# Moving steps between the slots of a hand-written order: attention steps, xr's splits, x2's splits and weight pieces

## The reference

```python
# attention, batch 8, heads 8, seq 576, head_dim 64, 32 packed queries
p_packed = softmax(p @ k.T / 8) @ v
x = softmax(q @ p_packed.T / 8) @ p_packed        # laid out as (8, 576, 512)
# first mixing layer, d_model 512, d_ff 1024
xk = mu_k * x + (1 - mu_k) * x_prev
xr = mu_r * x + (1 - mu_r) * x_prev
x2 = sigmoid(xr @ w_r) * (relu(xk @ w_k) ** 2 @ w_v)
# second mixing layer, rank 32, 4 * d_model = 2048
u = x2 + (x2.T @ U @ V).T
out = u + relu(u @ w_ch1) @ w_ch2
```

## Time and profile before

| what | us |
|---|---|
| median of 3 runs | 1340.4 (1338.31 to 1340.59) |
| the profiled execution | 1340.01 |
| its span | 1338.2 |
| TensorE busy | 1304.4 |
| VectorE busy | 957.9 |
| ScalarE busy | 697.1 |
| GpSimd busy | 233.5 |

### The profile page before, as it was taken

The page is one execution under the profiler, slowest core; times in us unless marked ns, Lnnn a source line. Parts: engine busy times, 40 slices in busy tenths (PEclk is TensorE's granted clock), DMA queues, the critical chain, the costliest instruction groups (busy, mean ns, idle before and its releaser), DMA issues.

```text
span 1338.2 us, 21378 instructions
## 1 busy us (share of the span) xinstructions
PE 1304.4 (97%) x7626; PEld 1128.1 (84%) x7626; DVE 957.9 (72%) x1557; ACT 697.1 (52%) x1233; POOL 233.5 (17%) x328
## 2 busy tenths in 40 slices
PE   7899999999999999999999999999999999999997
PEld 6768888878888888888999999888888888888886
DVE  5977978786878777774568676857587566857557
ACT  4657556456555555544546554645355534645353
POOL 3702132324142103511002003000030003000000
PEclk9999999999999999999999999999999999999999
DMA  9646595839384614965888899787757886678766
GB/s 241 160 76 107 124 177 128 161 101 175 81 173 106 156 24 123 286 189 132 276 271 253 271 267 314 237 248 218 233 187 197 258 225 213 192 207 215 220 194 136
DMA packets 431577, 252.57 MB, mean 189 GB/s; under 512 B 311536, under 2 KB 350480, under 8 KB 431472
## 3 DMA queue, kind: packets, MB, share of 16 engines
q1 hardware_dynamic: 414768, 232.31, 65.4%
q0 software_dynamic: 10096, 17.78, 4.9%
q10 hardware_dynamic: 6608, 1.11, 0.5%
HBM read 201.25 MB, written 49.81 MB: 188 GB/s over the span
## 4 chain that ended last, share of the span: by engine, by line
PE 75%; DVE 5%; SPq 4%; DMA 3%; issue 1%; ACT 1%; POOL 0%; DVEq 0%; ACTq 0%
PE bank L1178 25%; PE bank L1264 24%; PE bank L923 9%; PE bank L909 8%; PE bank L888 5%; SPq L1450 2%; DMA w_ring<-w_parts 1%; SPq L1588 1%; PE bank L1005 1%; PE bank L1077 1%; PE bank L713 1%; DMA kq_parts<-in_q 0%; DMA x_scratch<-x 0%; DVE square L972 0%; DVE x2s_lo L1016 0%
## 5 line engine op out<-in xcount | busy, mean ns | idle before, releaser
L1178 PE MATMUL bank<-u_parts,w_ring 128*128 128x512 f32 (+1 forms) x1680 | 353.7, 368 | 1.1 <-DVE hid_raw L1223 1.1
L1264 PE MATMUL bank<-hid_parts,w_ring 128*128 128x512 f32 (+1 forms) x1680 | 349.5, 368 | 1.2 <-DVE acc L1312 0.5
L1264 PEld LDWEIGHTS bank<-hid_parts,w_ring 128*128 128x128 f32 x1680 | 304.9, 188 | 44.2 <-issue 3.8
L1178 PEld LDWEIGHTS bank<-u_parts,w_ring 128*128 128x128 f32 x1680 | 304.9, 188 | 40.9 <-issue 1.8
L1287 ACT ACTIVATE hid_parts<-hid_raw 128x512 fp32r<-128x512 f32 (+1 forms) x280 | 164.7, 588 | 134.6 <-PE bank L1264 133.8
L1293 DVE TENSOR_TENSOR hid_parts<-hid_raw,hid_parts 128x512 fp32r<-128x512 f32 (+1 forms) x280 | 180.8, 646 | 63.5 <-ACT hid_parts L1287 59.0
L909 PE MATMUL bank<-xk_hi,wk_hi 128*128 128x384 f32 x384 | 132.1, 344 | 1.9 <-DVE x L983 1.9
L909 PE MATMUL bank<-xk_lo,wk_hi 128*128 128x384 f32 x384 | 129.5, 337 | 0.0
L909 PE MATMUL bank<-xk_hi,wk_lo 128*128 128x384 f32 x384 | 129.3, 337 | 0.0
L923 PE MATMUL bank<-wv_hi,k_hi 128*128 128x512 f32 x288 | 113.5, 394 | 0.0
L923 PE MATMUL bank<-wv_lo,k_hi 128*128 128x512 f32 x288 | 112.2, 390 | 0.0
(11 more groups left out here) (176 smaller groups left out, 1937.1 us busy)
## 6 DMA issues: line engine op xcount, KB each, us to landing
w_ring<-w_parts SPq DMA_DIRECT2D x560, 256.0 KB, 3.7
w_parts<-early_out SPq DMA_DIRECT2D x23, 896.0 KB, 5.0
x_scratch<-x SPq DMA_DIRECT2D x144, 64.0 KB, 2.1
kq_parts<-in_q SPq DMA_DIRECT2D x112, 72.0 KB, 2.9
w_parts<-piece_out SPq DMA_DIRECT2D x9, 896.0 KB, 4.6
kq_parts<-in_k SPq DMA_DIRECT2D x96, 72.0 KB, 4.0
x_tiles<-x_scratch SPq DMA_DIRECT2D x6, 1024.0 KB, 6.7
v_rows<-in_v POOLq DMA_DIRECT2D x41, 128.0 KB, 5.6
```

Of the source, the lines that this page charges most:

```text
L1178: last = nc.tensor.matmul(to, wring[:, e % RW, ct, a, :], uc[:, pos, b, ct, 0:w], start=(pos in FRESH and ct == 0 and a == 0 and b == 0), ...
L1264: last = nc.tensor.matmul(role(st, j, BANK_OF[pos])[:, 0:w], wring[:, e % RW, j, a, :], hid[:, no % RH, b, 0:w], start=(pos in FRESH and i ...
```

## The change

- FIRST_AT and EARLY_AT: early pieces move from 31, 38, 43 to 33, 39, 44 in the first group, and from 35, 39 to 36, 41 in the two middle groups.
- The batch whose plan is named fourth: norm1 from 50 to 51 and outA from 53 to 54 everywhere; pp from 40 to 41 and scores2 from 42 to 43 in the middle groups. Slot 51 is slot 0 of the next group, so norm1 comes to lie behind the chunk's border.
- Batch 1 in C0: pv and qA from slot 4 to 5, qB from 5 to 6.
- x2's split of slot 0 is placed ahead of the k tile's item instead of behind it. For TensorE nothing is changed by that; ScalarE and VectorE do the split before they wait for k0.
- xr's splits of the second and third chunk of a group (C2, C4, C5, C7, C8, C10, C11) move from slot 14 of the chunk before to slot 3 of their own chunk. C1 had its split at slot 4 of its own, and C0, C3, C6, C9 at slot 3 of their own, and keep it.
- In the last group the first four loads of pieces (ws_load) move from slot 6 to slot 4.

```diff
--- before.py
+++ after.py
@@ -69,7 +69,7 @@
 NG, NU = 2, 4
 NPROD = 7
 PIECES = 2 * 2 * NG * NU
-EARLY, FIRST_AT, EARLY_AT = 20, (23, 31, 38, 43), (1, 6, 11, 15, 27, 31, 35, 39)
+EARLY, FIRST_AT, EARLY_AT = 20, (23, 33, 39, 44), (1, 6, 11, 15, 27, 31, 36, 41)
 SLOTS_P = 3
 RW, RH = 11, 3
 MIX_AT = (9, 10, 12, 14)
@@ -100,14 +100,14 @@
 
     if kind == FIRST:
         third = batch_slots(15, 17, 20, 22, 23, 24, 25, 26, 28, 29, 31, 35, 36)
-        fourth = batch_slots(37, 38, 40, 42, 43, 44, 45, 46, 47, 49, 50, 53, 55)
+        fourth = batch_slots(37, 38, 40, 42, 43, 44, 45, 46, 47, 49, 51, 54, 55)
     else:
         third = batch_slots(6, 8, 11, 13, 15, 16, 17, 19, 21, 23, 25, 28, 30)
-        fourth = batch_slots(32, 33, 35, 37, 38, 39, 40, 42, 45, 47, 50, 53, 55)
+        fourth = batch_slots(32, 33, 35, 37, 38, 39, 41, 43, 45, 47, 51, 54, 55)
     here = (3, {at: steps for at, steps in fourth.items() if at < CHUNKS * NSLOT})
     rest = (1, {at - CHUNKS * NSLOT: steps for at, steps in fourth.items() if at >= CHUNKS * NSLOT})
     if kind == FIRST:
-        second = {0: ("scores1",), 2: ("a",), 4: ("pv", "qA"), 5: ("qB",), 8: ("pp",), 9: ("scores2",),
+        second = {0: ("scores1",), 2: ("a",), 5: ("pv", "qA"), 6: ("qB",), 8: ("pp",), 9: ("scores2",),
                   10: ("sm1", "norm0"), 11: ("norm1",), 13: ("outA",), 14: ("outB",)}
         return [(1, second), (2, third), here]
     return [rest, (2, third), here] if kind == MIDDLE else [rest]
@@ -133,14 +133,14 @@
     last_chunk = kind == LAST and c == CHUNKS - 1
     for at, slot in enumerate(SLOTS):
         s = c * NSLOT + at
+        if at == 0 and (c > 0 or kind != FIRST):
+            items.append(("x2s", 7 if c == 0 else 3 * c - 2, -1 if c == 0 else 0))
         items.append(slot)
         if at == (5 if c == 2 else 3) and (c > 0 or kind != FIRST):
             items.append(("x2s", 3 * c - 1, 0) if c > 0 else ("x2s", 8, -1))
         if c > 0 or kind != FIRST:
             behind = -1 if c == 0 else 0
-            if at == 0:
-                items.append(("x2s", 7 if c == 0 else 3 * c - 2, behind))
-            elif at == 2:
+            if at == 2:
                 items.append(("g", 7, 1, -1) if c == 0 else ("g", 3 * c - 2, 0, 0))
                 if c == 2:
                     items.append(("g_evac", 0, 0))
@@ -160,14 +160,14 @@
             items.append(("g", 3 * c, int(c == 2), 0))
         if not last_chunk:
 
-            at0 = (15, 15) if kind == FIRST and c == 0 else MIX_AT if c < 2 else MIX_AT[:3]
+            at0 = (15, 15) if kind == FIRST and c == 0 else MIX_AT[:3]
             for where, one in zip(at0, (("mix", 0), ("split", 0), ("mix", 1), ("split", 1))):
                 if at == where:
                     items.append(one + (c + 1,))
         if kind == FIRST and c == 1 and at in (2, 4):
             items.append(("mix" if at == 2 else "split", 1, 1))
-        if kind != FIRST and c == 0 and at == 3:
-            items.append(("split", 1, 0))
+        if at == 3 and (kind != FIRST or c == 2):
+            items.append(("split", 1, c))
         if kind == FIRST and c == 0 and at in (1, 3):
             items.append(("mix" if at == 1 else "split", 1, 0))
         if kind == FIRST and c == 0 and at in (2, 4):
@@ -223,7 +223,7 @@
 def piece_items():
 
 
-    plan = {6: [("ws_load", EARLY + m) for m in range(SLOTS_P + 1)]}
+    plan = {4: [("ws_load", EARLY + m) for m in range(SLOTS_P + 1)]}
     for m in range(PIECES - EARLY):
         n, at = EARLY + m, 9 + 9 * m // 5
         if 0 < m < PIECES - EARLY - SLOTS_P:
```

## The result

The changed kernel is slower. Its time is 1341.0 us (median of 20 runs) against 1338.4 for the kernel before in the runs beside it; the ratio is 1.0025, 95% interval 1.0016 to 1.0034, which is 2 to 4.5 us. The forecast was 1338.4 on a time before of 1340.4, a ratio of 0.9985.

A forecast was written before the change was run, and what follows sets the result against it. TensorE was taken to bound the kernel, busy 97% of the span, with its first-phase waits to win. The chunk terms summed to -1.85 us, giving 1338.2 or 1338.6, stated as 1338.4; range 1334.5 to 1342, to hold 8 in 10.

The forecast's parts named there:

- C4 and C7: Middle chunks: the split in slot 3, ahead of sm1, delays k5's relu and r0 by 0.55 each; +1.1 us, bounds 0 and +3.6.
- C10 and C11: Last group: the split delays relu5 in C10 and the sums for the u matmul in C11, 0.5 each; +1.0 us.
- the C10 wait of 1.1 stays: Expected in the profile after: TensorE's wait of 1.1 us in C10 remains.
- C2: First group: the 1.88 wait for x and probably the half rate go, new waits take some back; -1.9 us.
- C3: x2's low part goes ahead of k0, removing a 0.84 wait, but outA's copy comes later for outB; 0 us.
- C6 and C9: The same reorder of x2's split, norm1 and outA where no wait was: +0.2 and +0.05; bounds 0 and +1.5.
- C5 and C8: pp one slot later, behind k7, so its 1.27 wait for packed goes; -1.4 us each, -2.8 together.
- C0: pv behind k5 loses its 1.42 wait, but relu5 holds r0 and scores2 comes up to 0.5 later; +0.5 us.
- Rival 4: New waits in front of outB in C2 and C3 tip TensorE's clock to half rate: 1341.5 us, chance 0.05.
- rival 2: The slot 3 split delays TensorE in full in C4, C7, C10, C11; C5 and C8 gain 0: +5.95, 1346; chance 0.15.
- three signs of being wrong: No L888 wait in C4 and C7; L689 still waiting in C5; C0's pv wait coming back as gain at 73.50.

The follow-up runs named there:

- scores2 without outA: The kernel with pp and scores2 one slot later in C5 and C8, plus C0's scores2, sm1, norm0 and norm1 one slot later: 0.9992 of the kernel before.
- the one with a single line of it: The kernel before with only pp and scores2 one slot later in C5 and C8 (40 to 41, 42 to 43): ratio 0.9963, 1332.8 us.
- C0 alone: The kernel before with only batch 1's pv, qA and qB one slot later in C0: ratio 1.0014.
- the last one: The changed kernel without the moves of xr's splits and without C0's moves: ratio 0.9979 of the kernel before, 1334.3 us.

## Why the prediction was wrong

The step that failed is the price of the splits' arrival. The prediction has for C4 and C7 "Slots 8 to 13 follow with slack. +1.1", and for C10 and C11 "+1.0". Measured between the two profiles: +2.9 and +2.4, and close to it in the kernel with the splits alone (+2.7 and +2.0). The first wait was as worked out with the earlier trace rows: r0 was to start 0.55 later, and starts 0.53 later in both. What I did not follow was the same delay one bank further: norm0 and k7's square on VectorE, then k7's high part and the sigmoid's table load on ScalarE, stand between the split and r0's evacuation, and v0 wants that bank. So the sum lacks a term that it put at nothing ("with slack"): TensorE idles 0.44 and 0.58 more in front of v0, and with the first matmuls behind each wait 0.9 and 1.0 come on top of the 0.53. In C10 the relu was 0.95 late, not 0.5, and the wait on x2s_lo, of which the prediction says that "the C10 wait of 1.1 stays", grew to 1.70. It is 1.2 to 1.7 in the four kernels with C10's split in slot 1 or 3 and 0.6 to 1.1 in the eight others. In the three with slot 3 ScalarE stood 3.9 to 4.4 for GpSimd's sum, in those eight 3.4 to 3.7; why is open. In C11 the wait for the sums grew by 0.8, not 0.5.

The other steps, in the prediction's order:

- C2: forecast -1.9, found -1.4. The 1.88 wait and the half rate went; the new waits stood where they were put: outB on L823 (forecast 1.1, found 0.87) and scores1 on the key transposes (forecast 0.7, found 1.13). The splits alone gave -1.8 there. Part of it is the state of the one execution: with the old order and full rate C2 is 53.0, not 53.8. So the end of the half rate is worth 0.8 by itself, and not the 1.65 of its matmuls, since at full rate outB waits 0.68 for its copy.
- C3: forecast 0, found -0.2; the wait at outB was forecast at 1.3 and is 0.81. Right.
- C6 and C9: +0.25 forecast, +0.8 found in this pair. Over the six kernels with this reorder C6 is 0.2 to 0.8 longer and C9 0.1. Right in kind, too small for this pair.
- C5 and C8: -2.8 forecast, -3.0 found. VectorE's packed began at 315.60 in C5 and pp at 316.93, without a wait. Right.
- C0: +0.5 forecast, +1.0 found, and +1.3 between the means of the four kernels with the new order (54.7 to 57.2) and the seven with the old (54.3 to 55.9), which overlap. The wait in front of r0 was named, but I let it end there: the clock fell behind it, and r0's 12 matmuls took 4.4 us instead of 2.8. Rival 4 had the mechanism, at the wrong places.

The sum of the forecast's chunks was -1.85, found +2.6 from the phase's first k tile on; of the 4.4 us between them 3.2 are the four chunks of the splits. So rival 2's mechanism decided it in the four chunks, at 5.3 of the 7.1 us that it had for them. Its total of +5.95 was more than twice the +2.6 found, mostly since C5 and C8, which it let gain nothing, kept their 3.0. The range of 1334.5 to 1342 held the time itself, and that was luck: the kernel before took 1338.4 in the runs beside it and not 1340.4, and on the prediction's own base the ratio of 1.0025 would be 1343.8. The direction was wrong, and the chance of 0.15 for "slower" too low: five terms (C2, C4 and C7, C6, C10 and C11, C0) rested on a slack of about the size of the thing put into it, and all their errors pointed one way. None of its three signs of being wrong came: the one for C4 and C7 looked at the first wait behind the split, and not at the second.

## What to carry to other kernels

A VectorE step cost here by where it stood in the list: nothing in slot 1 of C4 and C7, 1.4 and 1.5 us in slot 3. Before moving one, follow the delay through every bank that rotates behind it, past the first one that waits, until a gap of that engine is larger than the step. Moving a TensorE step behind one more tile wins its wait only if its own successors keep their distance (pp with scores2 did, scores2 without outA did not). Judge an order edit of a few us by the lengths of the stages in the profile where these repeat better than whole runs, look at the granted clock before reading a difference in one that does not, and test the edit's parts alone: here no version measured faster than the one with a single line of it.

## What the runs showed of the hardware

The same wait is followed by half rate in one execution and not in the next. TensorE waited 2.40 to 2.48 us for packedT in C0 in nine kernels; the matmuls behind it ran at half rate (r tiles 0.43 us apart) in five of them, the kernel before, the changed one, the splits alone (there from scores2 itself on), C0 alone and the last one, and at full rate (0.23 apart) in the other four. These rows are of pp and scores2 alone, to be set beside the earlier trace rows:

```profile
73.51 1.20 PE L700 MATMUL bank<-kqT,packedT 64*32 64x288 f32 x32 [2.48 <-ACT packedT L733]
...
75.21 0.40 PE L888 MATMUL bank<-wr_hi,xr_lo 128*128 128x512 f32 x1
75.44 0.40 PE L888 MATMUL bank<-wr_hi,xr_hi 128*128 128x512 f32 x1
```

The wait for x in C2 behaves alike: half rate behind it in the kernel before (1.88) and in C0 alone (1.66), full rate in pp and scores2 alone (1.89) and two others (1.87, 1.88). So the length of a wait alone does not tell what follows: 1.66 was followed by half rate and 2.48 by full. A change that brings a wait of that size can buy a stretch at 1.2 GHz in some executions. Such a stretch cost TensorE about 1.5 to 1.7 us here (an estimate from the starts in the rows), of which 0.8 was left in the length of C2 and 1.6 in that of C0 (55.9 against 54.3). That it is part of the scatter between runs of one kernel is likely and not shown, since only one execution of each was profiled.
